# VectorE's softmax steps in other places of the loop, and three score tiles at the start of an attention and two-layer kernel

## What is computed

```python
kv_pool = kv.reshape(B, H // r, r, W // r, r, C).mean(axis=(2, 4))   # r = 4, 768 windows
kv_flat = kv_pool.reshape(B, -1, C) @ w_sr
k = v = kv_flat
s = scale * (q @ k.transpose(0, 2, 1))        # 12288 queries, C = 128
s = s - s.max(-1, keepdims=True)
a = np.exp(s)
a /= a.sum(-1, keepdims=True) + 1e-09
x = a @ v
# first network, d_ff = 2048
h = x @ w_in
g = np.where(h >= 1, h, np.where(h <= -1, 0.0, (h + 1) ** 2 / 4))
y = g @ w_out
# second network, d_ff = 2048
h = y @ w_in2
out = (h / (1.0 + np.exp(-1.702 * h))) @ w_out2
```

## Time and profile before

| what | us |
|---|---|
| median of 3 runs (lowest, highest) | 1370.16 (1368.46, 1370.78) |
| the profiled execution, by the device's clock | 1368.36 |
| its span in the trace | 1366.5 |
| TensorE busy (share of the span) | 1273.1 (93%) |
| VectorE busy | 1074.2 (79%) |
| ScalarE busy | 1027.4 (75%) |
| GpSimd busy | 986.5 (72%) |

### The profile page before, as it was taken

One profiled execution on the slowest core, in us unless ns is written; L12 is line 12 of the kernel. 1 busy time (PEld: TensorE's weight loads), 2 busy tenths in 40 slices (PEclk: granted clock), 3 DMA queues, 4 the chain that ended last, 5 costly groups with the idle time before them and its releaser, 6 DMA issues.

```text
span 1366.5 us, 17127 instructions
## 1 busy us (share of the span) xinstructions
PE 1273.1 (93%) x5496; PEld 1033.6 (76%) x5496; DVE 1074.2 (79%) x1234; ACT 1027.4 (75%) x1083; POOL 986.5 (72%) x411
## 2 busy tenths in 40 slices
PE   5468999999999999999999999999999999999988
PEld 3345778787787787787787877877877878778866
DVE  6889887887888878878878888788788788876433
ACT  3656777787777787787778777877887787787666
POOL 2636687696696786876966967968769769679770
PEclk9879999999999999999999999999999999999999
DMA  9100010001000000100000000001000000000000
GB/s 332 39 16 16 9 32 17 15 15 31 15 15 19 27 15 15 31 15 15 19 27 15 15 25 22 15 15 31 15 15 27 20 16 8 24 16 1 16 8 16
DMA packets 18605, 36.19 MB, mean 26 GB/s; under 512 B 3344, under 2 KB 3472, under 8 KB 18320
## 3 DMA queue, kind: packets, MB, share of 16 engines
q1 hardware_dynamic: 18576, 35.83, 8.1%
HBM read 29.43 MB, written 6.39 MB: 26 GB/s over the span
## 4 chain that ended last, share of the span: by engine, by line
PE 62%; DVE 16%; issue 9%; ACT 5%; POOL 5%; DMA 2%; SPq 0%; DVEq 0%; ACTq 0%; POOLq 0%
PE ps_ring L343 12%; PE ps_ring L345 12%; PE ps_ring L344 12%; PE ps_y L343 9%; PE ps_y L345 9%; PE ps_y L344 9%; DVE s_sb L701 5%; POOL g_lo L306 3%; DVE g_hi L751 2%; DVE g L758 2%; POOL g_lo L313 2%; ACT g L586 2%; DVE row_sum L723 2%; ACT g_hi L572 2%; ACT g L579 1%
## 5 line engine op out<-in xcount | busy, mean ns | idle before, releaser
L313 POOL TENSOR_TENSOR g_lo<-g,g_hi 128x1024 fp32r<-128x1024 f32 x192 | 505.7, 2634 | 174.2 <-DVE g L758 174.2
L306 POOL TENSOR_TENSOR g_lo<-g,g_hi 128x1024 fp32r<-128x1024 f32 x181 | 437.0, 2414 | 134.8 <-ACT g_hi L572 77.0
L751 DVE SCALAR_TENSOR_TENSOR g_hi<-g,ps_ring 128x1024 fp32r<-128x1024 f32 x192 | 234.1, 1219 | 176.3 <-ACT g L586 176.3
L570 ACT ACTIVATE g<-ps_ring 128x1024 f32<-128x1024 f32 x192 | 197.3, 1028 | 172.9 <-PE ps_ring L345 172.6
L343 PE MATMUL ps_y<-g_hi,w_hi 128*128 128x512 f32 x768 | 301.7, 393 | 14.7 <-POOL g_lo L313 12.1
L345 PE MATMUL ps_y<-g_hi,w_lo 128*128 128x512 f32 x768 | 299.6, 390 | 0.0
L344 PE MATMUL ps_y<-g_lo,w_hi 128*128 128x512 f32 x768 | 299.5, 390 | 0.0
L758 DVE SCALAR_TENSOR_TENSOR g<-g,ps_ring 128x1024 f32<-128x1024 f32 x192 | 232.9, 1213 | 0.0
L586 ACT ACTIVATE g<-g 128x1024 f32<-128x1024 f32 x192 | 204.5, 1065 | 5.4
L579 ACT ACTIVATE g<-ps_ring 128x1024 f32<-128x1024 f32 x192 | 197.9, 1030 | 13.8 <-POOL g_lo L313 7.3
L572 ACT ACTIVATE g_hi<-ps_ring 128x1024 fp32r<-128x1024 f32 x192 | 195.7, 1019 | 5.1 <-PE ps_y L345 5.1
(11 more groups left out here) (69 smaller groups left out, 1739.3 us busy)
## 6 DMA issues: line engine op xcount, KB each, us to landing
kv_sb<-in_kv_t SPq DMA_DIRECT2D x12, 512.0 KB, 8.2
q_sb<-in_q_t SPq DMA_DIRECT2D x24, 256.0 KB, 3.7
key_max<-max_row SPq DMA_DIRECT2D x24, 256.0 KB, 3.4
inv_sum<-inv_row SPq DMA_DIRECT2D x24, 256.0 KB, 3.2
out_t<-y_sb SPq DMA_DIRECT2D x24, 256.0 KB, 3.5
w_raw<-in_moe_w_in SPq DMA_DIRECT2D x2, 1024.0 KB, 17.2
max_row<-max_turned SPq DMA_DIRECT2D x24, 2.0 KB, 1.3
inv_row<-inv_turned SPq DMA_DIRECT2D x24, 2.0 KB, 1.3
```

What stands on the lines that cost most here:

```text
L306: nc.gpsimd.tensor_tensor(g2_lo[:, slot, :], g2[:, slot, :], g2_hi[:, slot, :].bitcast(F32), ALU.subtract).then_inc(g2_lo_done, 1)
L313: nc.gpsimd.tensor_tensor(g1_lo[:, slot, :], g1[:, slot, :], g1_hi[:, slot, :].bitcast(F32), ALU.subtract).then_inc(g1_lo_done, 1)
L570: nc.scalar.activation(g2[:, slot, :], ps_h2(k), ACT.Gelu_apprx_sigmoid).then_inc(g2_done, 1)
L751: nc.vector.scalar_tensor_tensor(out=g1_hi[:, uu % 2, :], in0=g1[:, uu % 2, :], scalar=1.0, in1=ps_h1(k), op0=ALU.min, op1=ALU.max).then_i ...
```

## The change

In the loop, on VectorE: `add_keys` of pair 1 moves from step 5 to 3, of pair 2 from step 5 to 4; `shift` of pair 1 from step 6 to 5, of pair 2 from step 7 to 6; `invert` from step 6 to 5. In `invert` the epsilon is added by a tensor_tensor with a constant tile `eps` in place of a tensor_scalar.

```diff
-                    if k == 6:
+                    if k == 5:
                         shift(it, half, 1)
-                    if k == 7:
+                    if k == 6:
                         shift(it, half, 2)
                 if is_tile(it - 1):
                     if k == 3:
                         add_keys(it - 1, 1 - half, 0)
-                    if k == 5:
                         add_keys(it - 1, 1 - half, 1)
+                    if k == 4:
                         add_keys(it - 1, 1 - half, 2)
-                    if k == 6:
+                    if k == 5:
                         invert(it - 1)
...
-                nc.vector.tensor_scalar(row, row, 1e-9, None, ALU.add).then_inc(eps_added, 1)
+                nc.vector.tensor_tensor(row, row, eps[:, :], ALU.add).then_inc(eps_added, 1)
```

```diff
+            def w_upper(m):
+                pool.wait_ge(w_loaded[m], 16)
+                for p in range(WP):
+                    cols = slice((m * WP + p) * WCH, (m * WP + p + 1) * WCH)
+                    nc.gpsimd.tensor_copy(w_hi[:, cols], w_raw[:, cols]).then_inc(w_hi_done[m], 1)
...
             def block_of_chunks(it):
+                if is_number(it, 3):
+                    for c in range(KC):
+                        score_chunk(it, c)
+                    return
...
-            for t in range(2):
+            for t in range(3):
                 for c in range(KC):
                     score_chunk(t, c)
             for c in range(KC):
                 value_chunk(2, c)
+            step(2, 0, 2)
+            step(2, 0, 3)
             for c in range(KC):
-                score_chunk(2, c)
-            for k in range(U):
+                value_chunk(3, c)
+            for k in range(4, U):
                 step(2, 0, k)
...
+            sp.wait_ge(summed, 9)
+            sp.dma_start(q2_sb[:, :], q_t[:, 2 * T:3 * T]).then_inc(q2_loaded, 16)
...
-            load_q(2)
             spread_max(0)
+            spread_max(1)
             load_q(3)
+            load_q(4)
             spread_inv(0)
-            spread_max(1)
-            load_q(4)
             spread_inv(1)
             spread_max(2)
```

More of the change, by code:

```diff
@@ L64, in encoder_kernel @@
         g1_hi = sb(ctx, "g1_hi", [P, 2, UW], F32R)
+        with ExitStack() as ramp:
+            key_max1 = sb(ramp, "key_max1", [P, T])
         g1_lo = sb(ctx, "g1_lo", [P, 2, UW], F32R)
+        with ExitStack() as ramp:
+            q1_hi = sb(ramp, "q1_hi", [C, T], F32R)
+            q1_lo = sb(ramp, "q1_lo", [C, T], F32R)
+            q2_hi = sb(ramp, "q2_hi", [C, T], F32R)
+            q2_lo = sb(ramp, "q2_lo", [C, T], F32R)
+            q2_sb = sb(ramp, "q2_sb", [C, T])
+            s_third = sb(ramp, "s_third", [P, KC, T])
         g2 = sb(ctx, "g2", [P, 2, UW])
@@ L110, in encoder_kernel, with is_number, ps_o, s_keys @@
         ps_y2 = ps(ctx, "ps_y2", [P, T])
+        def is_number(t, number):
+            return isinstance(t, int) and t == number
         def ps_s(c):
             return ps_ring[:, 0, (c % 2) * T:(c % 2 + 1) * T]
-        ps_o = ps_ring[:, 1, 0:T]
+        def ps_o(t):
+            return ps_y2[:, :] if is_number(t, 1) else ps_ring[:, 1, 0:T]
+        def s_keys(t, slot, chunks):
+            return s_third[:, chunks, :] if is_number(t, 2) else s_sb[:, slot, chunks, :]
         def ps_h2(k):
@@ L553, in probs_upper @@
                 at_least(act, pv_done, (t - 1) * KC + (2 * p + 2))
-                copy(pt_hi[:, 2 * p:2 * p + 2, :], s_sb[:, slot, 2 * p:2 * p + 2, :]).then_inc(pt_hi_done, 1)
+                copy(pt_hi[:, 2 * p:2 * p + 2, :], s_keys(t, slot, slice(2 * p, 2 * p + 2))).then_inc(pt_hi_done, 1)
             def x_upper(t, half):
@@ L594, in iteration @@
             def iteration(it, half):
+                if is_number(it, 3):
+                    x_upper(1, 1)
+                    for c in range(KC):
+                        evacuate(3, 1, c)
                 if is_tile(it - 1):
@@ L599, in iteration @@
                         probs_upper(it - 1, 1 - half, p)
-                if is_tile(it - 2):
+                if is_tile(it - 2) and not is_number(it, 3):
                     x_upper(it - 2, half)
@@ L609, in _ @@
             v_upper(1)
-            evacuate(0, 0)
-            q_upper(1, 1)
-            w_upper(0)
-            evacuate(1, 1)
-            q_upper(2, 0)
+            evacuate(0, 0, 0)
+            evacuate(0, 0, 1)
+            act.wait_ge(q_loaded, 32)
+            copy(q1_hi[:, :], q_sb[:, 1, :]).then_inc(q_hi_done, 1)
+            evacuate(0, 0, 2)
+            evacuate(0, 0, 3)
+            act.wait_ge(q2_loaded, 16)
+            copy(q2_hi[:, :], q2_sb[:, :]).then_inc(q_hi_done, 1)
+            evacuate(0, 0, 4)
+            evacuate(0, 0, 5)
+            for c in range(KC):
+                evacuate(1, 1, c)
+            for c in range(KC):
+                evacuate(2, 0, c)
             for p in range(PAIRS):
@@ L699, in shift @@
                 dve.wait_ge(max_spread, t * 16 + 16)
-                pair = s_sb[:, slot, 2 * p:2 * p + 2, :]
-                nc.vector.tensor_tensor(pair, pair, key_max[:, :].unsqueeze(1).to_broadcast([P, 2, T]),
+                row = key_max1 if is_number(t, 1) else key_max
+                pair = s_keys(t, slot, slice(2 * p, 2 * p + 2))
+                nc.vector.tensor_tensor(pair, pair, row[:, :].unsqueeze(1).to_broadcast([P, 2, T]),
                                         ALU.subtract).then_inc(shifted, 1)
@@ L782, in step @@
                         shift(it, half, 0)
+                    if k == 5:
+                        shift(it, half, 1)
                     if k == 6:
-                        shift(it, half, 1)
-                    if k == 7:
                         shift(it, half, 2)
```

195 lines of the change are left out of this document (105 added, 90 removed).

## The result

Before: 1369.3 us median of 4 runs (1368.4 to 1370.8). Changed: **1348.9 us** median of 4 runs (1348.1 to 1349.5). The ratio is 0.985, 95% interval 0.983 to 0.987. The change makes the kernel 20 us faster. The forecast was 32 us, and 1347 was the upper end of the forecast range. The profiled execution of the changed kernel has a span of 1347.6 us, against 1366.5 before: 18.9 less.

The account below looks back on a forecast made before the run. TensorE was taken to set the 53.56 us period, waiting once per iteration for VectorE's late score copies. Savings of 28.5 (loop), 2.5 (ramp) and 1.2 (end) make 32.2 us, giving 1337 us, range 1329 to 1347.

Parts of the forecast that it names:

- 51.65: TensorE's matmul work per loop iteration, in us: 228 matmuls of 0.2265, the base of the predicted period of 52.05.
- The part on steps 3 to 7: VectorE's reorder in the loop: only one of `invert`'s instructions changes, period falls to 52.05, saving 28.5 us.
- The gap closes: At the loop's third score chunk: VectorE's copies start 2.9 us earlier, ending TensorE's wait with 1.3 to spare.
- Shift 1 takes its turn and the epsilon line waits: VectorE in the loop: shift 1 waits for GpSimd, 509.5 to 511.8; the epsilon line waits too, taking 1.17 us.
- A new wait of 0.25 for `g2_lo` of unit 6: TensorE's layer-out in each loop iteration waits 0.25 us for GpSimd's operation, whose slack of 1.1 is used up.
- no new wait: Rival: in the loop g2_lo comes just in time, period 51.75 to 51.8, 37.5 us saved, time 1332; chance 0.20.
- The ramp, 2.5: Before the loop: third score chunk of iteration 4 at 145.4 instead of 147.90, 2.5 us gained, range -5 to +5.
- The stations: Ramp waypoints: casts 1.2 us, first layer-in at 64.05, scores of iteration 3 at 91.2, next layer-in at 109.6.
- The end, 1.2: Iteration 24: TensorE's wait of 0.82 for unit 7 of tile 23 and slow restart of 0.3 vanish, gaining 1.2 us.

Follow-up runs that it names:

- fourth kernel: Changed kernel with the epsilon buffer placed behind all others, so x, y1 and inv_sum lie where they lay before: 1337.1 us.
- first kernel: Kernel before plus only the epsilon buffer, ahead of inv_sum, x and y1, and the tensor_tensor that reads it: 1378.3 us.
- eighth kernel: Changed kernel, epsilon buffer last, ScalarE's first Gelu of iteration 3 no longer behind VectorE's third sum (wait moved to the second Gelu): 1332.2 us.
- second kernel: Kernel before with only the new order of VectorE's steps 3 to 7; no new buffer, old ramp: 1338.4 us.
- tenth: Against the eighth kernel: 256 unused bytes ahead of inv_sum, so inv_sum, x and y1 lie 256 bytes further: 1331.0 us.
- third: Changed kernel with the old order of VectorE's steps from iteration 4 on; new ramp and epsilon buffer stay: 1377.4 us.
- eleventh: Against the eighth kernel: 128 unused bytes ahead of w_hi, so every tile lies 128 bytes further: 1329.8 us.
- ninth: Against the eighth kernel: 64 unused bytes ahead of w_hi, so every tile lies 64 bytes further: 1333.2 us.
- fifth: Changed kernel with the epsilon buffer 32 columns wide, so inv_sum, x and y1 lie 128 bytes further than before: 1346.8 us.
- sixth: Changed kernel with the epsilon buffer between x_lo and y1_hi: x in its old place, y1 64 bytes further: 1345.6 us.
- seventh: Changed kernel with the epsilon buffer between inv_sum and x_sb and a gap ahead of y1: x 64 bytes further than before, y1 128: 1350.7 us.
- twelfth: Against the eighth kernel: k_hi, k_lo, v_hi and v_lo 64 bytes further, everything behind them 256 bytes further: 1335.4 us.

## Why the prediction was wrong

Its range ended at 1347; the time was 1348.9. **The step that failed is the first term of the sum: "51.65", 228 matmuls of 0.2265 each, carried over from the trace of before into the changed kernel.** The part on steps 3 to 7 says that no instruction is added or removed, which holds, and the epsilon line was costed as an operation of VectorE, at 0.16 to 1.17 us in VectorE's slack. Its buffer was costed nowhere. By the fourth kernel that buffer is 19 x (52.43 - 51.87) = 10.6 us of the loop and 2.5 of the stretch behind iteration 23 (204.2 against 201.7). The steps alone stretch by 8 x (5.53 - 5.44) = 0.7 us per iteration (sums of the table's rows); the period shows 0.56, as the longer steps also hide a short wait (third point below).

The other steps, in the changed kernel and, where the long step covers them, in the fourth:

- **The gap closes**: right. The copies start at 512.10, as soon as VectorE is through with `g1_hi` of unit 7; the first is done by 512.7, and TensorE writes the ring half at 514.31, 1.6 later (1.3 predicted). VectorE's rows of the same step as the earlier trace rows:

```profile
502.24 2.24 DVE L765 TENSOR_TENSOR s_sb<-s_sb,key_max 128x1024 f32<-128x1024 f32 x1
...
505.61 1.16 DVE L787 TENSOR_TENSOR row_sum<-row_sum,eps 32x16 f32<-32x16 f32 x1
...
509.63 1.22 DVE L765 TENSOR_TENSOR s_sb<-s_sb,key_max 128x1024 f32<-128x1024 f32 x1
510.96 1.22 DVE L815 SCALAR_TENSOR_TENSOR g_hi<-g,ps_ring 128x1024 fp32r<-128x1024 f32 x1
512.10 1.28 DVE L731 COPY s_sb<-ps_ring 128x512 f32<-128x512 f32 x2
```

- **Shift 1 takes its turn and the epsilon line waits** (2.3 and 1.17 predicted): 2.24 and 1.16. The form with two inputs saves nothing: a median of 1162 ns over 24, where the old form had 1152. Their minima, 1151 and 161, don't set them apart: in the old ramp one of the 24 meets GpSimd just as it ends, and there the new form too takes 161 (first kernel).
- **A new wait of 0.25 for `g2_lo` of unit 6**: right in kind, too large. In the changed kernel it does not come: GpSimd is through at 509.11, TensorE starts the group at 509.53. In the fourth kernel, with TensorE at its old step, it comes in every iteration, at the place foretold. The list of waits on matmuls misses it, as the records of two matmuls overlap; the weight load shows it:

```profile
503.54 2.42 POOL L334 TENSOR_TENSOR g_lo<-g,g_hi 128x1024 fp32r<-128x1024 f32 x1
...
505.81 0.39 PE L379 MATMUL ps_y<-g_hi,w_lo 128*128 128x512 f32 x1
506.01 0.19 PEld L377 LDWEIGHTS ps_y<-g_hi,w_hi 128*128 128x128 f32 x1 [0.24 <-POOL g_lo L334]
506.04 0.48 PE L377 MATMUL ps_y<-g_hi,w_hi 128*128 128x512 f32 x1
506.35 0.40 PE L378 MATMUL ps_y<-g_lo,w_hi 128*128 128x512 f32 x1
```

The weight load sits idle for 0.24, but the step of the matmuls is 0.31 in place of 0.23: the wait costs 0.08 to 0.09. A second one of 0.11, in every other iteration, was there before (596.68, 703.80). So the period is 228 x 0.2267 + 0.09 + 0.05 = 51.83 of the 51.87 measured; 52.05 was forecast, 51.75 to 51.8 by the rival "no new wait". Loop gain in the fourth kernel 32.1, forecast 28.5.
- **The ramp, 2.5**: 0.6, and 0.3 in the fourth kernel. The stations were near: casts 1.04 to 1.07 (1.2), first layer-in 62.66 (64.05), scores of iteration 3 at 90.37 (91.2), the layer-in after them at 107.29 (109.6). What is missing is the stall at 132.26. The wait that makes it is in the diff, and the working went past it: it did not ask who is queued behind the waiting Gelu. The eighth kernel without it comes to 143.63, where 145.4 was predicted. Differences of 0.3 to 0.6 are themselves no more than chance here: the first score matmul, which the change hardly touches, starts at 22.34 to 23.45 over these kernels.
- **The end, 1.2**: 0.8 in the second and tenth kernels (200.2 behind the third score chunk of iteration 23, against 201.0). In the changed kernel and the fourth it was a loss, by the long step in the first and by the clock in both (below).

The fourth kernel's 1337.1 is the predicted 1337, but by two errors that cancel, 3.6 too little for the loop and 4 too much for ramp and end: the agreement is luck.

## What to carry over

Costing a change by instructions and waits leaves out one of its effects: a new buffer moves all that are allocated behind it. Keep tiles that meet in a matmul at the same place modulo 256 bytes, as every fast layout here has them, put small buffers last, and after any edit of the allocations compare the mean step of matmuls without a wait between them, that of the groups behind the suspected one too. And where buffers share memory, read from each new wait what is queued behind it, and let each instruction wait only for the part that it overwrites.

## What the runs showed of the hardware

**The step of a matmul depends on where its tiles lie.** With 128x512 matmuls of three passes, back to back at full clock, the mean step is 0.2266 to 0.2277 when all operand tiles start at the same place modulo 256 bytes, and 0.229 to 0.234 in the groups that read a tile 64 or 128 bytes off. It holds for a moved streaming operand (x, y1) and for moved weights (k, v). The slowness goes on behind the last such group: ten matmuls at 64 bytes and three at 128 for x and y1, six for k and v. The Trainium skill, page "SBUF — State Buffer", section "Operand start alignment", asks only for a start at a multiple of the element size and says that its runs "timed nothing"; all layouts here keep that rule. Open: why it goes on, and why longer at 64 bytes than at 128. No run moves only tiles that other engines use, so that the relation is the one between streamed tile and weights is the plainest reading and not shown apart. Other offsets were not tried. The cause inside the chip was not measured.

**The clock after the same wait.** In the last iterations TensorE waits 2.3 to 2.4 us for VectorE. In the second kernel's profiled execution it restarts at full clock and stays there:

```profile
1282.81 0.50 PE L343 MATMUL ps_ring<-y_hi,w_hi 128*128 128x512 f32 x1 [2.35 <-DVE g L758]
1283.14 0.39 PE L344 MATMUL ps_ring<-y_lo,w_hi 128*128 128x512 f32 x1
```

In that of the changed kernel three steps of 0.23 to 0.35 are followed by seven of 0.43, at half clock:

```profile
1292.63 0.51 PE L377 MATMUL ps_ring<-y_hi,w_hi 128*128 128x512 f32 x1 [2.29 <-DVE g L822]
1292.98 0.40 PE L378 MATMUL ps_ring<-y_lo,w_hi 128*128 128x512 f32 x1
...
1293.48 0.63 PE L377 MATMUL ps_ring<-y_hi,w_hi 128*128 128x512 f32 x1
1293.90 0.63 PE L378 MATMUL ps_ring<-y_lo,w_hi 128*128 128x512 f32 x1
```

The granted clock of 10 us around it is 1.00 in the one (1280 to 1290 us) and 0.83 in the other (1290 to 1300), a mix of 2.4 and 1.2 GHz. The third, fourth, eighth and eleventh kernels have such a stretch too, and the ninth has two; the kernel of before and the first, second, fifth, sixth, seventh, tenth and twelfth have none. It costs 1.4 us: the two waits for VectorE are 15.04 us apart in the fourth kernel and 13.61 in the second. What decides it was not found; so a term of this size at a wait of 2.3 us can't be forecast from one trace.
